# Another order of the attention steps on four engines, y kept in x's channel layout, and a head of 20 slots instead of 22

## The reference

```
mag = sqrt(a_re^2 + a_im^2);  scale = min(mag, 0.999) / (mag + 1e-06);  (a_re, a_im) *= scale
for t in range(S):
    S_re, S_im = ar*S_re - ai*S_im + k[t] v[t]^T,  ar*S_im + ai*S_re
    y[t] = q[t] . S_re
x = y as (tokens, heads * 48)
h = x @ w_in;   x = max(0.01 h, h) @ w_out
h = x @ w2_in;  out = where(h > 0, h, exp(min(h, 0)) - 1) @ w2_out
```

## Time and profile before

| | |
|---|---|
| device time, median of 3 runs | 1178.68 us (1177.75 to 1183.27) |
| the profiled execution | 1179.06 us, its span 1177.4 us |
| TensorE matmul, busy | 1051.5 us (89%) |
| VectorE, busy | 732.8 us (62%) |
| ScalarE, busy | 606.4 us (52%) |
| DMA, share of 16 engines | 20.7% |
| ScalarE table loads (L275) | 51, 65.4 us |

### The profile page before, as it was taken

How to read it: one execution, slowest core, us unless ns; L and a number is a source line. 1 busy time by engine, 2 the same in 40 slices (tenths; PEclk the granted TensorE clock), 3 DMA queues, 4 the chain that set the end, 5 groups by cost and what they waited for, 6 DMA issues and landing times.

```text
span 1177.4 us, 17157 instructions
## 1 busy us (share of the span) xinstructions
PE 1051.5 (89%) x6312; PEld 936.2 (80%) x6312; DVE 732.8 (62%) x1459; ACT 606.4 (52%) x1152; POOL 1.9 (0%) x15
## 2 busy tenths in 40 slices
PE   1455887889899999999999999999999999999996
PEld 1355777878777887877878889999999999999995
DVE  4766777677877787778776334664444445454442
ACT  6656667676666676677664334642333323233321
POOL 0000000000000000000000000000000000000000
PEclk9997899899999999999999999999999999999998
DMA  5343222332222222233211003420101001010000
GB/s 100 101 104 84 55 42 47 67 62 41 41 62 41 44 70 44 53 62 68 41 28 41 14 2 108 127 81 1 54 1 54 1 2 54 1 54 1 28 1 30
DMA packets 163722, 56.23 MB, mean 48 GB/s; under 512 B 129968, under 2 KB 159792, under 8 KB 163632
## 3 DMA queue, kind: packets, MB, share of 16 engines
q1 hardware_dynamic: 163632, 55.08, 20.7%
HBM read 40.89 MB, written 9.44 MB: 43 GB/s over the span
## 4 chain that ended last, share of the span: by engine, by line
PE 67%; ACT 14%; DVE 13%; issue 5%; DMA 0%; DVEq 0%; SPq 0%; ACTq 0%
PE ph L726 25%; PE acc L744 22%; PE even L744 4%; PE odd L821 3%; ACT L275 2%; PE odd L800 2%; PE even L812 2%; PE even L800 2%; DVE qk L573 2%; PE even L814 2%; PE chain L752 1%; ACT sq L337 1%; ACT sq L335 1%; DVE ang L521 1%; DVE sines L569 1%
## 5 line engine op out<-in xcount | busy, mean ns | idle before, releaser
L302 ACT CAST g_hi<-gf 128x512 fp32r<-128x512 f32 (+2 forms) x208 | 122.5, 589 | 307.7 <-DVE gf L471 136.8
L726 PE MATMUL ph<-x_hi,win_hi 128*128 128x512 f32 (+2 forms) x624 | 234.9, 377 | 5.3 <-DVE x_lo L622 3.3
L726 PE MATMUL ph<-x_lo,win_hi 128*128 128x512 f32 (+2 forms) x624 | 235.4, 377 | 0.0
L726 PE MATMUL ph<-x_hi,win_lo 128*128 128x512 f32 (+2 forms) x624 | 235.3, 377 | 0.0
L480 DVE TENSOR_TENSOR g_lo<-gf,g_hi 128x512 fp32r<-128x512 f32 (+2 forms) x208 | 134.3, 645 | 129.7 <-ACT g_hi L302 129.7
L294 ACT ACTIVATE gx<-ph 128x512 f32<-128x512 f32 (+2 forms) x208 | 116.7, 561 | 117.9 <-PE ph L726 117.8
L726 PEld LDWEIGHTS ph<-x_hi,win_hi 128*128 128x128 f32 x624 | 118.8, 190 | 24.3 <-issue 6.6
L726 PEld LDWEIGHTS ph<-x_hi,win_lo 128*128 128x128 f32 x624 | 118.4, 190 | 19.1
L726 PEld LDWEIGHTS ph<-x_lo,win_hi 128*128 128x128 f32 x624 | 118.6, 190 | 16.7
L744 PE MATMUL acc<-g_hi,wout_hi 128*128 128x512 f32 (+2 forms) x336 | 130.6, 389 | 0.0
L744 PE MATMUL acc<-g_lo,wout_hi 128*128 128x512 f32 (+2 forms) x336 | 122.8, 365 | 0.0
(11 more groups left out here) (133 smaller groups left out, 1680.4 us busy)
## 6 DMA issues: line engine op xcount, KB each, us to landing
wraw<-in_moe_w_in SPq DMA_DIRECT2D x32, 192.0 KB, 2.5
wraw<-in_moe_w_out SPq DMA_DIRECT2D x32, 192.0 KB, 2.7
ar<-in_a_re SPq DMA_DIRECT2D x24, 192.0 KB, 3.2
ai<-in_a_im SPq DMA_DIRECT2D x24, 192.0 KB, 3.7
qk<-in_q SPq DMA_DIRECT2D x24, 192.0 KB, 4.2
qk<-in_k SPq DMA_DIRECT2D x24, 192.0 KB, 4.4
vs<-in_v SPq DMA_DIRECT2D x24, 192.0 KB, 4.2
rot<-hidden SPq DMA_DIRECT2D x6, 768.0 KB, 5.8
```

The costliest lines, as they stand in the source:

```text
L302: sc.copy(gs[0][:, n % 2, 0:size], gf[:, n % 2, 0:size]).then_inc(g_hi, 1)
L726: ins = mm(ph[n % 2][:, 0:size], win[hi][:, j, kc], xs[lo][:, T % 2, kc, 0:size], start=i == 0, stop=i == KC * len(PARTS) - 1)
```

## The change

It has five parts.

1. **Order.** The lists of steps in a slot are placed anew on TensorE, VectorE, ScalarE and SyncE. Some steps get another slot too: `inverse` 4 to 1, `tangents` and `gains` 5 to 4, `angles` 6 to 5, `angles_across` 7 to 6, `load_gates` -1 to -2, `load_v` 7 to 8.
2. **Channels of y.** x's channels get another order: partitions 32g to 32g + 31 of the first block hold channels 0 to 31 of head g, of the second block those of head 4 + g, and of the third block the last 16 channels of heads 2g and 2g + 1. v is loaded in that layout with zeros between (DP = 64 columns per head), y comes out of TensorE in x's layout, `w_in` of layer 0 is loaded with its rows in that order, and `chunk_to_x` reads the bank itself in offset 14. `yt`, `xraw`, `y_columns` and `to_channels` are gone.
3. **HEAD** is 20 instead of 22.
4. **Weight splits** of layer 0 are in the slots of the list W0_SLOTS instead of slots 8 to 23.
5. **Guards.** The three reductions are replaced by accumulator outputs of two ScalarE activations that are there anyway; the two squares of a chunk's gates become one over 768 columns.

```diff
-    HEAD, WLAG, XSTEP, WS, TB = 22, 3, 4, 2, TOK // P
+    HEAD, WLAG, XSTEP, WS, TB = 20, 3, 4, 2, TOK // P
+    W0_SLOTS = (8, 9, 11, 13, 15, 16, 17, 18, 19, 21, 22, 23, 24, 26, 27, 30)
...
         def weight_at(a):
-            j = a - (HEAD - 14)
-            if 0 <= j < FC:
-                return j
+            if a in W0_SLOTS:
+                return W0_SLOTS.index(a)
...
-                sp.dma_start(vs[:, m % 2], v[b, :, c * P:(c + 1) * P, :].rearrange("h t d -> t h d")) \
-                    .then_inc(in_v[m % 2], 16)
+                else:
+                    sp.wait_ge(pads_ready, 1)
+                vt = v[b, :, c * P:(c + 1) * P, :].rearrange("h t d -> t h d")
+                sp.dma_start(vs[:, m % 2, :, 0:DA], vt[:, :, 0:DA]).then_inc(in_v[m % 2], 16)
+                for r in range(2):
+                    sp.dma_start(vs[:, m % 2, r::2, DA + r * DB:DA + (r + 1) * DB], vt[:, r::2, DA:]) \
+                        .then_inc(in_v[m % 2], 16)
...
-            def y_columns(m):
-                act.wait_ge(y_made, m + 1)
-                if m:
-                    act.wait_ge(x_in[(m - 1) % 2], 160 * ((m - 1) // 2 + 1))
-                sc.activation(yt[0:112].rearrange("p h t -> p (h t)"), even[0:112, :], ACT.Copy,
-                              scale=0.25).then_inc(y_out, 1)
-
             def chunk_to_x(m):
                 T = tile_of(m)
                 tok = m * P - tiles[T][1]
-                act.wait_ge(x_in[m % 2], 160 * (m // 2 + 1))
+                act.wait_ge(y_made, m + 1)
                 if T >= 2:
                     act.wait_ge(h_made, (T - 1) * FC)
-                sc.copy(xs[0][:, T % 2, :, tok:tok + P], xraw[:, m % 2]).then_inc(x_hi, 1)
+                sc.activation(xs[0][:, T % 2, :, tok:tok + P], even[:, 0:E].rearrange("p (c t) -> p c t", c=KC), ACT.Copy,
+                              scale=0.25).then_inc(x_hi, 1)
...
-                for p in range(HP):
-                    for r in range(2):
-                        h = 2 * p + r
-                        o = even[64 * r:64 * r + D, p * P:(p + 1) * P]
-                        ins = mm(o, vs[:, m % 2, h], scm[:, h], start=True, stop=first(m))
-                        if not first(m):
-                            ins = mm(o, state[:, h], qd[:, h], start=False, stop=True)
+                for c in range(2):
+                    for g in range(4):
+                        h = 4 * c + g
+                        ins = mm(even[DA * g:DA * (g + 1), c * P:(c + 1) * P], vs[:, m % 2, h, 0:DA], scm[:, h], start=True,
+                                 stop=first(m))
+                    for g in range(4 if not first(m) else 0):
+                        h = 4 * c + g
+                        ins = mm(even[DA * g:DA * (g + 1), c * P:(c + 1) * P], state[:, h, 0:DA], qd[:, h], start=False,
+                                 stop=True)
+                for r in range(2):
+                    for g in range(4):
+                        h = 2 * g + r
+                        ins = mm(even[DA * g:DA * (g + 1), 2 * P:3 * P], vs[:, m % 2, h, DA:], scm[:, h], start=r == 0,
+                                 stop=r == 1 and first(m))
...
             for a in range(SLOTS):
+                if (m := chunk_at(a, 8)) is not None:
+                    decay_back(m)
+                if (m := chunk_at(a, 13)) is not None:
+                    scores(m)
...
```

More of the change, by code:

```diff
@@ L650, in _ @@
                     square_sum(m)
+                if (x := x_step_at(a)) is not None:
+                    split_x(*x)
+                if (m := chunk_at(a, 4)) is not None:
+                    tangents(m)
                 if (m := chunk_at(a, 10)) is not None:
                     turns(m)
+                if (m := chunk_at(a, 15)) is not None and not end(m):
+                    next_state(m)
+                if (m := chunk_at(a, 7)) is not None:
+                    ends(m)
+                if chunk_at(a, 17) == M - 1:
+                    judge()
@@ L653, in _ @@
+                if chunk_at(a, 19) == M - 1:
+                    verdict()
+                if (n := item_at(a, 1)) is not None:
+                    from_h(n)
+                if (m := chunk_at(a, 8)) is not None:
+                    scale_by_decay(m)
+                if (m := chunk_at(a, 14)) is not None and not end(m):
+                    sum_state(m)
+                if (m := chunk_at(a, 7)) is not None:
+                    phases(m)
                 if (m := chunk_at(a, 13)) is not None:
@@ L827, in judge @@
                 pe.wait_ge(sine_ready, M)
-                for i in range(3):
+                for i in range(2):
                     mm(chain[0:1, i * P:(i + 1) * P], worst[:, i:i + 1], ident[:], start=True, stop=True)
-                mm(chain[0:1, 3 * P:3 * P + D2], worst[0:D2, 3:4], ident[0:D2, 0:D2], start=True,
+                mm(chain[0:1, 2 * P:2 * P + D2], worst[0:D2, 2:3], ident[0:D2, 0:D2], start=True,
                    stop=True).then_inc(worst_t, 1)
```

268 lines of the change are left out of this document (115 added, 153 removed).

## The result

The changed kernel takes **1081.05 us** (median of 4 runs, 1079.82 to 1083.36) where the kernel before takes 1178.86 (4 runs, 1177.75 to 1183.27): a ratio of 0.917, interval 0.914 to 0.920. The profiled execution took 1079.82 us, its span is 1078.0.

A forecast was written before the change was run, and what follows sets the result against it. Waits through the engines bound head and tile 0, TensorE mostly the rest. Up to tile 6, 80 + 87 + 90 + 306 + 83 = 646 against 709.7 us; 1179.06 - 63.7 = 1115.4, forecast 1115 us, range 1095 to 1140 (1150 with pairs).

The forecast's parts named there:

- Rivals A: In y's products only pairs of passes overlap, +1.76 us a chunk, +35 us in all, 1150 us; chance 10%.
- C: In y's products 32-column passes don't overlap at all, 5.1 us a chunk, +108 us, 1223 us; chance 4%.
- for which I take 34: Head: two half-filled rounds before round four's gains' transpose, 31.4 us by ratio, taken as 34; summed 15.3 + 34 + 21.
- 12 us for copies and slots and 14 for the order: Head: split of its gain from 106.3 to 80 us between removed copies and two slots, and the new order.
- up to 5 us a round, of which I count half, since items now sit between the steps: Tile 0: the head's three cuts shorten its rounds too; 24.0 - 2.3 = 21.7 us a round, four times 87 us.
- VectorE's fill being 81%: Tile 0: share of its 87 us in which VectorE, with 70.7 us of work, would be busy, instead of 73%.
- at least 87 us of TensorE: Tile 1: TensorE's busy 91.2 us at clock 0.95, taken at the full clock as a floor; forecast 90 us.
- the gains' hole: Tiles 2 to 4: TensorE's 0.47 us wait before the gains' transpose, to go since gains were made two slots ahead.
- the phases' hole: Tiles 2 to 4: TensorE's 1.06 us wait before the phases' transpose, to go since the scores now stand there.
- `up` runs before it (2 us more for the scaling): Tiles 2 to 4: up ahead of the phases' transpose gives VectorE's scaling 2 us more, part of the 306 us forecast.
- Rival B: Waits move and don't go: new holes of 1.5 us a round, tiles 0 to 4 unchanged, 1164 us; chance 9%.
- Tile 5 (83: Tile 5: two slots less ahead put half a round's attention, 4.25 us, beside items, less a hole; 79.6 becomes 83 us.

The follow-up runs named there:

- ygroup: The changed kernel with y's passes issued two of a group of 32 output columns in a row; y's first row to the next product took 3.29 us, after 1.90.
- gates_late: The changed kernel with inverse, tangents, gains, angles and angles_across back in their old slots; this cost 33.6 us.
- layout_old_order_20: The kernel with the new layout of y, direct way to x and guards without reductions, HEAD 20, but the old order and slots of steps; 1163.9 us.
- reductions_4: The changed kernel with four unused reductions over 384 columns a chunk added on VectorE; head 7.5 us longer, tile 0 4.9, tile 1 1.6, tiles 2 to 4 nothing.
- scores_late: The changed kernel with TensorE's scores behind up and the phases' transpose, as before; 1088.7 us.
- scans_late: The changed kernel with VectorE's scans of the decays behind turns and from_h, as before, instead of first in the slot; 1092.9 us.
- decay_late: The changed kernel with decay_back and the second columns step behind up again on TensorE; tiles 2 to 4 took 299.7 us, and the place was worth nothing in all.
- gates_alone: layout_old_order_20 with only the gate steps in their new slots and the gain scan at the head of VectorE's row; 1177.3 us.
- gates_pe: The kernel of gates_alone with TensorE's whole row in the new order, the other engines' rows otherwise left as there; 1122.1 us.

## Why the prediction was too slow

**y (right).** 1.8 us a chunk, starting in fours. Rivals A (pairs) and C (none overlap) are out, and with them the only slower case. The Trainium skill, "TensorE: Matmul & The Clock Gate", Part 3, has matmuls start and end in strict order. Of the starts the rows say otherwise (the ends are modelled): in ygroup all four groups' L787 start from 364.98 us on, ahead of the first group's L791 at 365.22, which the program issues second; in the kernel after four passes of different groups start 7 ns apart. The factor of 4 of the Trainium skill, "TensorEngine Tiling (Array Packing)", Theoretical Speedup, agrees with the rows (64 passes of 0.11 us in 1.8).

**Head (80, measured 68.8).** "for which I take 34": the first three terms were each too long. The start at 15.3 was taken as fixed, and the order moved it to 11.4 (-3.9, of which gates_late shows 3.8 to be the gates' place); the first two rounds took 31.8 us, near the 31.4 that the ratio gave and that I had raised to 34; round three took 19.6 instead of 21; and from slot 18 to the first product came 6.1 us instead of 9.5, since the states (1.49 us) and y run at the fast level there: y is read 3.9 us after the gains' transpose, and I had left the 7.2 us of the slow level. My split of the head's gain, 12 us for copies and slots and 14 for the order, came out as 13.8 (layout_old_order_20, 92.5) and 23.7: the order's part was mis-sized.

**Tile 0 (87, measured 77.0).** The failed step is "up to 5 us a round, of which I count half, since items now sit between the steps", the largest error beside the head's. The round fell from 24.0 to 19.25 us, so nearly the whole 5 us came; counted in full, the term gives 4 x 19.0 = 76 us. "VectorE's fill being 81%" failed with it: the fill is 95%. The lower bound of 79 us was too high as well. VectorE's sum, 70.7 us in the forecast and 73.4 in the trace, is the floor near which the time came to lie, and reductions_4 shows that it matters; scores_late (82.5 us), scans_late (80.4) and gates_late (83.0) show that the order has to be right for the tile to get there.

**Tile 1 (90, measured 83.9).** The "at least 87 us of TensorE" was no floor, as the 83.9 us for the same items and more passes show. My reading of why: TensorE's busy time holds the modelled end of each pass (at 408.83 us a pass of 0.39 us is followed by the next start 0.23 us later), so it shrinks when passes close up.

**Tiles 2 to 4 (306, measured 299.6).** The total was 6 us off by the same error (303.7 us busy was no floor either). Of the two reasons that I gave, one held: gates_late brings the gains' hole back (11.6 us). The other is not borne out. The scores' place alone is not what ended the phases' hole (scores_late), and "`up` runs before it (2 us more for the scaling)" misread the lists: up preceded that transpose in the old order too, and the 2 us would come from `decay_back`, which now stands ahead of its own slot's up; alone, that is not needed either (decay_late). What the runs do show is that the gates' slots took half of the phases' waits and TensorE's new row the rest (gates_alone, gates_pe), that the two gate transposes need room between them (gates_apart), and that the last wait goes with the rows of the other engines. Rival B, the waits that move, is out; gates_alone shows that it was a real danger: two steps in one slot that share a buffer made a new wait of 1.55 us, larger than either hole that was there.

**Tile 5 (83, measured 80.9) and the rest (469.4, measured 469.6)** stand. The errors, -11.2, -10.0, -6.1, -6.4, -2.1 and +0.2, sum to -35.6 us, which is the difference between the forecast (1115.4) and the profiled execution (1079.8). All of a sign: I took the round of each stage from the old round less named cuts, with half of a cut kept as room for what may be late next. Nothing of weight came late next, and from tile 0 on the stages went down to their fullest engine.

## What to carry to other kernels

When an order of steps is laid out anew, forecast each stage with its work on the fullest engine as the lower end (here VectorE at 95%, TensorE at 100%), and with the old round less the whole cuts as the upper end. In a stage where no engine is full, as in the head (ScalarE 81%), the chain of waits has to be summed instead. Parts of an order don't add up: the same five slot numbers were worth -13 us alone, and 34 when taken out of the finished order; look for steps in a slot that write one buffer and put other work between them. Sum starts of passes, not their lengths, for what TensorE needs.

## What the runs showed of the hardware

- fp32 passes of 32 output columns in four groups run four at a time, 27.5 ns a pass, and overtake waiting passes of other groups, as if each group held one running and three waiting; eight in a row for one group stop the others (3.29 instead of 1.90 us to the next product).
- TensorE's clock rose and fell within the head. In the kernel after, four passes of the decays' transpose took 0.55 us at 52.95 and the scores' eight 2.08 at 57.09 (1.16 at the fast level); the gains' transpose took 1.06 us at 43.18 and 0.61 at 62.75, the levels of 1.2 and 2.4 GHz. The clock column gives 0.95 for the whole head. Idle products between steps brought the fast level (1.16 against 2.07 us) and only 2.5 us of time.
- An accumulated output of ScalarE comes with an instruction of its own, 0.18 to 0.19 us (ACTIVATION_READ_ACCUMULATOR).
- GpSimd's subtractions (1.0 us and more against VectorE's 0.55) lengthened VectorE's operations on two tensors beside them (0.56 to 1.14, 0.94 to 1.56 us), and small ones of 96x4 most of all (means of 0.15 and 0.16 to 0.69 and 0.67 us).
